# Decayed-attention stage of a fused attention and two-layer expert kernel: 64x64 array tiles for two products, a two-step state update, and two smaller moves

## The reference

```python
def _attn_ref(r, k, v, w, u) -> np.ndarray:
    B, H, S, D = r.shape                     # 4, 8, 768, 48
    state = np.zeros((B, H, D, D), dtype=np.float32)
    y = np.zeros_like(r)
    for t in range(S):
        kt, vt, rt = (k[:, :, t], v[:, :, t], r[:, :, t])
        cur = np.einsum('bhd,bhe->bhde', u[None] * kt, vt)
        y[:, :, t] = np.einsum('bhd,bhde->bhe', rt, state + cur)
        state = w[None, :, :, None] * state + np.einsum('bhd,bhe->bhde', kt, vt)
    return y.astype(np.float32)
...
    x = np.ascontiguousarray(attn_out.transpose(0, 2, 1, 3)).reshape(B * S, H * D)
    x = _moe_ref(x=x, **moe_kwargs)           # 8 experts, 384 of 3072 tokens each: relu(x @ w1[e]) @ w2[e]
    return _moe2_ref(x=x, **moe2_kwargs)      # relu(x @ w_in)**2 @ w_out, width 2048
```

## Time and profile before

| | us |
|---|---|
| median of 3 runs | 817.01 |
| lowest and highest of the runs | 812.26 and 819.65 |
| the profiled execution, as a run | 811.83 |
| its span in the profile | 810.1 |
| TensorE busy in the span | 775.9 (96%) |
| attention's units, TensorE: first `scores` to the last gate | 7.6 to 127.3 |

### The profile page before, as it was taken

One profiled execution on the slowest core, in us unless ns is written; L12 is line 12 of the kernel. 1 busy time (PEld: TensorE's weight loads), 2 busy tenths in 40 slices (PEclk: granted clock), 3 DMA queues, 4 the chain that ended last, 5 costly groups with the idle time before them and its releaser, 6 DMA issues.

```text
span 810.1 us, 19168 instructions
## 1 busy us (share of the span) xinstructions
PE 775.9 (96%) x6971; PEld 741.8 (92%) x6971; DVE 501.4 (62%) x1195; ACT 321.4 (40%) x718; POOL 293.5 (36%) x295
## 2 busy tenths in 40 slices
PE   7999995789999999999999999999999999999996
PEld 6999994589899999999999999999999999999995
DVE  7888886787846783678377837783777236721210
ACT  4555654223532353235323532353236324531332
POOL 8666640102631263126312631263126312621333
PEclk9999996699999999999999999999999999999999
DMA  8888744502300140013001300130013002300000
GB/s 215 240 257 242 230 141 177 167 18 77 110 1 30 48 137 0 29 54 131 0 29 57 128 0 29 57 127 0 29 59 125 0 30 79 108 1 30 0 1 30
DMA packets 22196, 65.27 MB, mean 81 GB/s; under 512 B 3664, under 2 KB 6736, under 8 KB 22160
## 3 DMA queue, kind: packets, MB, share of 16 engines
q1 hardware_dynamic: 19088, 55.34, 21.6%
q0 software_dynamic: 3072, 9.44, 3.3%
HBM read 55.33 MB, written 9.44 MB: 80 GB/s over the span
## 4 chain that ended last, share of the span: by engine, by line
PE 76%; DVE 12%; issue 5%; POOL 3%; ACT 2%; DMA 1%; POOLq 0%; DVEq 0%; SPq 0%; ACTq 0%
PE bank L1359 14%; PE bank L1363 14%; PE bank L1360 13%; PE bank L1417 7%; PE bank L1418 6%; PE bank L1419 6%; PE bank L1163 3%; PE bank L1201 3%; PE bank L1176 3%; DVE hot L860 2%; DVE hot L974 2%; PE bank L1230 1%; DVE sq L1073 1%; PE bank L1217 1%; POOL xg L473 1%
## 5 line engine op out<-in xcount | busy, mean ns | idle before, releaser
L500 POOL TENSOR_TENSOR h_lo<-sq,h_hi 128x384 fp32r<-128x384 f32 x128 | 155.4, 1217 | 375.7 <-DVE sq L1073 375.6
L1073 DVE SCALAR_TENSOR_TENSOR sq<-bank,relu 128x384 f32<-128x384 f32 x128 | 71.1, 555 | 150.4 <-ACT relu L624 148.4
L624 ACT ACTIVATE relu<-bank 128x384 f32<-128x384 f32 x128 | 62.9, 492 | 193.6 <-PE bank L1363 180.3
L1417 PE MATMUL bank<-m_hi,h_hi 128*128 128x384 f32 x384 | 132.2, 344 | 2.3 <-POOL h_lo L500 2.0
L1359 PE MATMUL bank<-x_hi,m_hi 128*128 128x384 f32 x384 | 129.6, 337 | 0.6
L1363 PE MATMUL bank<-x_hi,m_lo 128*128 128x384 f32 x384 | 130.0, 338 | 0.0
L1418 PE MATMUL bank<-m_lo,h_hi 128*128 128x384 f32 x384 | 129.6, 338 | 0.0
L1419 PE MATMUL bank<-m_hi,h_lo 128*128 128x384 f32 x384 | 129.2, 337 | 0.0
L1360 PE MATMUL bank<-x_lo,m_hi 128*128 128x384 f32 x384 | 128.8, 335 | 0.0
L618 ACT ACTIVATE h_hi<-bank 128x384 fp32r<-128x384 f32 x64 | 31.5, 492 | 175.4 <-PE bank L1363 175.4
L1065 DVE SCALAR_TENSOR_TENSOR h_lo<-bank,h_hi 128x384 fp32r<-128x384 f32 x64 | 35.5, 554 | 73.2 <-ACT h_hi L618 73.2
(11 more groups left out here) (191 smaller groups left out, 1446.5 us busy)
## 6 DMA issues: line engine op xcount, KB each, us to landing
w_raw<-we_in SPq DMA_DIRECT2D x48, 512.0 KB
nn<-nn_in SPq DMA_DIRECT2D x24, 384.0 KB, 3.9
tt<-tt_in SPq DMA_DIRECT2D x44, 192.0 KB, 4.3
m_raw<-m_in SPq DMA_DIRECT2D x12, 512.0 KB, 6.3
x_rows<-yrow SPq DMA_DIRECT2D x24, 192.0 KB, 2.4
tt<-tt_in SPq DMA_DIRECT2D x4, 256.0 KB, 5.7
xg<-x_rows,perm_next POOLq DMA_INDIRECT x24, 5.3
out<-xg,perm_now POOLq DMA_INDIRECT x24, 2.6
```

Source lines behind the costliest of these rows:

```text
L500: pool.tensor_tensor(h_lo[g % 3][:, :], sq[g % 2][:, :], h_hi[g % 3][:, :].bitcast(f32), ALU.subtract).then_inc(lo2_ready, 1)
L624: act.activation(relu[:, :], h_ps[g % 3][:, 0:CAP], ACT.Relu).then_inc(relu_ready, 1)
L1073: dve.scalar_tensor_tensor(out=sq[g % 2][:, :], in0=h_ps[g % 3][:, 0:CAP], scalar=0.0, in1=relu[:, :], op0=ALU.max, op1=ALU.mult).then_inc ...
L1417: pe.matmul(acc_ps[t][:, 0:DM], h_hi[r][:, s], m2_hi[:, c:c + DM], start=first, stop=False)
```

## The change

- `scores` and `inter` are cut by 64 also in the other direction: `scores` computes 64 columns of weights (64 of the 128 key steps) at a time into half of the partitions, and `inter` 64 of the 128 query steps. Each has 16 products where it had 8. `inter` streams 64 columns of the state where it streamed 128 (48 are used), and the padding of `state` shrinks with it. In front of both, TensorE raises a semaphore of its own (`pe_held`), so that the waits stand in its instruction stream ahead of the products and not in the first weight load.
- `state_sum` becomes one multiplication of the state by `w_chunk` into a new tile `faded`, which stands in front of the waits for `update_ready` and `inter_done`, and one addition of the PSUM result, which also waits for `faded_ready`.
- `in_high` rounds half a tile (512 columns) behind each of the last two units of a chunk; the semaphore counts two per tile, and the waits for it are doubled.
- GpSimd waits for `scaled` to reach 3 before it makes `rk` of unit 2, once.

```diff
-        state = [sb(f"state{b}", [HD, PAIRS * D + P - D], f32, att) for b in range(B)]
+        state = [sb(f"state{b}", [HD, PAIRS * D + HALF - D], f32, att) for b in range(B)]
+        faded = sb("faded", [HD, PAIRS * D], f32, att)
...
-                        sp.wait_ge(in_hi_ready, i + 1)
+                        sp.wait_ge(in_hi_ready, 2 * i + 2)
...
             def in_low(i, part):
-                pool.wait_ge(in_hi_ready, i + 1)
+                pool.wait_ge(in_hi_ready, 2 * i + 2)
...
+                    if is_first(i) and b == 0:
+
+                        pool.wait_ge(scaled, 3)
                     if not last or b < B - 2:
                         bonus(i + (b + 2) // B, (b + 2) % B)
...
-            def in_high(n):
+            def in_high(n, piece):
                 act.wait_ge(in_loaded, 16 * n + 16)
-                cols = bass.ds(n * WT, WT)
+                cols = bass.ds(n * WT + piece * (WT // 2), WT // 2)
...
-                    if not last and b == B - 1:
-                        in_high(i + 1)
+                    if not last and b >= B - 2:
+                        in_high(i + 1, b - B + 2)
...
             def state_sum(i, b):
                 n = 4 * i + b
+                dve.wait_ge(state_ready, n + B)
+                dve.tensor_tensor(faded[:, :].rearrange("p (q d) -> p q d", q=PAIRS),
+                                  state[b][:, 0:PAIRS * D].rearrange("p (q d) -> p q d", q=PAIRS),
+                                  w_chunk[:, :].unsqueeze(2).broadcast_to([HD, PAIRS, D]), ALU.mult).then_inc(faded_ready, 1)
                 dve.wait_ge(update_ready, n + 1)
                 dve.wait_ge(inter_done, n + 1)
-                for p in range(PAIRS):
-                    c = slice(p * D, (p + 1) * D)
-                    done = dve.scalar_tensor_tensor(out=state[b][:, c], in0=state[b][:, c], scalar=w_chunk[:, p:p + 1],
-                                                    in1=u_ps[0:HD, c], op0=ALU.mult, op1=ALU.add)
-                done.then_inc(state_ready, 1)
+                dve.wait_ge(faded_ready, n + 1)
+                dve.tensor_tensor(state[b][:, 0:PAIRS * D], faded[:, :], u_ps[0:HD, 0:PAIRS * D],
+                                  ALU.add).then_inc(state_ready, 1)
...
             def scores(i, b):
+                pe.sem_inc(pe_held, 1)
                 for p in range(PAIRS):
                     for a in range(2):
                         rows = slice(a * HALF, a * HALF + D)
-                        last = pe.matmul(sc_ps[a][:, p * P:(p + 1) * P], ks[rows, p, :], rs[j][rows, p, :], start=True, stop=True)
+                        for s in range(0, P, HALF):
+                            last = pe.matmul(sc_ps[a][s:s + HALF, p * P:(p + 1) * P], ks[rows, p, s:s + HALF], rs[j][rows, p, :],
+                                             start=True, stop=True)
...
             def inter(i, b):
+                pe.sem_inc(pe_held, 1)
                 for p in range(PAIRS):
                     for a in range(2):
                         rows = slice(a * HALF, a * HALF + D)
-                        last = pe.matmul(y_ps[j][:, a, p * P:(p + 1) * P], rs[j][rows, p, :], state[b][rows, p * D:p * D + P],
-                                         start=p == 0, stop=False)
+                        for t in range(0, P, HALF):
+                            last = pe.matmul(y_ps[j][t:t + HALF, a, p * P:p * P + HALF], rs[j][rows, p, t:t + HALF],
+                                             state[b][rows, p * D:p * D + HALF], start=p == 0, stop=False)
```

More of the change, by code:

```diff
@@ L244, in build @@
         rk_ready, own_made, ownv_ready = sem("rk_ready"), sem("own_made"), sem("ownv_ready")
-        kn_ready, state_ready = sem("kn_ready"), sem("state_ready")
+        kn_ready, state_ready, faded_ready = sem("kn_ready"), sem("state_ready"), sem("faded_ready")
         yT_sum, yT_ready, logit_sum, logit_ready = sem("yT_sum"), sem("yT_ready"), sem("logit_sum"), sem("logit_ready")
@@ L256, in build @@
         perm_kept = sem("perm_kept")
-        pool_held = sem("pool_held")
+        pool_held, pe_held = sem("pool_held"), sem("pe_held")
         gather_sent = sem("gather_sent")
@@ L577, in units @@
                         own_values(i + (b + 1) // B, (b + 1) % B)
-                    if not last and b == B - 1:
-                        in_high(i + 1)
+                    if not last and b >= B - 2:
+                        in_high(i + 1, b - B + 2)
             own_copy(0, 0)
             own_values(0, 0)
-            in_high(0)
+            in_high(0, 0)
+            in_high(0, 1)
             units(0, False)
```

## The result

| | before | after |
|---|---|---|
| median of 20 runs of each, us | 814.85 | 822.25 |
| lowest and highest, us | 811.34 and 822.68 | 816.22 and 835.06 |
| ratio after to before | | 1.0078 (95%: 1.0053 to 1.0102) |
| profiled execution, us, and its span | 811.8, 810.1 | 821.4, 819.6 |
| `scores` of unit 8 starts at, us | 47.39 | 58.29 |

The forecast was 810 in a range up to 820: wrong, and on the other side. The three stretches (+10.9, -3.7, +1.8 us) give 9.0 of the 9.5 us by which the spans differ. So the change won in the middle most of what was promised (0.29 us a unit for 0.36), and lost three times as much in the first eight units.

What follows compares the result with a forecast made beforehand. TensorE was taken as the bound, 4.745 us per unit going to 4.39. Start -1.0, 18 units -6.4, `pe_held` +0.5 and tail 0 gave -6.9 us: 817.0 - 7 = 810 us, range 801.5 to 820.

Steps and rivals of the forecast that it cites:

- the start: First units of the attention: `scores` of unit 3 starts earlier, -1.0 us in the sum, bounds -1.7 and 0.
- The tail: Last three units of the attention: TensorE alone would win 1.3 us, but VectorE enters late; taken as 0.
- Scores and inter in four tiles: TensorE's products: four tiles run at once, `inter` 0.45 us for 0.89, `scores` 1.06, saving 0.44 us per unit on `inter`.
- The slow rival: TensorE still runs only two tiles at a time: `scores` over 1.5 us, unit +0.9, total 834 us; chance 0.13.
- State sum: VectorE's `faded` stands behind GpSimd's `kn` in some units, making 4.39 us per unit; bounds 4.25 and 4.7.
- `pe_held`, "between 0 and 0.1 us per unit": Waits ahead of TensorE's products cost nothing when running ahead, a restart when `rs` is just in time; taken as 0.03.
- Weights in halves: ScalarE's halved weight copy no longer holds back `yT` in one unit of four: 0.05 us per unit, 0.9 us in all.
- rk of unit 2 later: GpSimd: `rs` of unit 2 takes 0.7 us instead of 2.44; after later meetings -1.0 us remains.
- DMA: Input transfers: same bytes in less time, share 0.90, inputs requested four units ahead; costed at nothing.
- The sum: Whole attention: start -1.0, 18 units -6.4, `pe_held` +0.5, last three units 0; together -6.9 us.
- The clock: Attention: a granted clock below full would show the forecast wrong; no sign of it seen, no chance given.

Runs made afterwards that it cites:

- e2: The changed kernel with the four old state operations in place of `faded` and the addition; 818.59 us, ratio 1.0033 to the kernel before.
- e13: e11 plus the change's two `pe_held` increments per unit on TensorE's queue, old tiles; 817.85 us, ratio 1.0001 to the kernel before.
- e8: The kernel before with only GpSimd's later `rk` of unit 2 added; 812.29 us, ratio 0.9966 to the kernel before.
- e12: The changed kernel without the later `rk` of unit 2; 822.18 us, ratio 1.0083 to the kernel before.
- e6: The changed kernel, but in the last chunk GpSimd waits for the unit's row sum before multiplying `rk`; 823.90 us, ratio 1.0066 to the kernel before.
- e1: The changed kernel with `scores` back to its old products, only `inter` in four tiles; 818.07 us, ratio 0.9991 to the kernel before.
- e17: The changed kernel without `pe_held`, each group's first product in old form, old state operations, old tiles in units 0 to 3; 827.04 us, ratio 1.0115.
- e14: e7 with the change's GpSimd order and `pe_held` only ahead of `inter`, from unit 4 on; 812.50 us, ratio 0.996 to the kernel before.
- e18: e14 with `scores` in four tiles too from unit 4 on, `pe_held` ahead of both; 814.14 us, ratio 0.9973 to the kernel before.
- e3: The changed kernel loading only a quarter of each input of units 4 to 23; 820.34 us, ratio 1.0034 to the kernel before.
- e11: e8 plus ScalarE's weight copies in two halves, all else old; 811.62 us, ratio 0.9942 to the kernel before.
- e4: The kernel before loading only a quarter of each input of units 4 to 23; 814.69 us, ratio 0.999 to the kernel before.
- e10: e8 plus the state sum as two operations (`faded`, addition), tiles unchanged; 815.37 us, ratio 0.999 to the kernel before.
- e7: The changed kernel with `scores` in halves, old tiles in units 0 to 3, old state operations, `rk` after the row sum in the last chunk; 815.76 us, ratio 0.9972.
- e9: e8 plus 64 bare semaphore increments per unit on TensorE's queue; 1108.86 us, ratio 1.3608 to the kernel before.
- e15: The changed kernel without `pe_held`, the first product of `scores` and of `inter` in old form; 832.22 us, ratio 1.0113 to the kernel before.

## Why the prediction was wrong, step by step

The step that failed is the start, -1.0 us in the sum: it measured +10.9. TensorE waited for its own program, which the prediction counted neither in bytes nor in time, and ran at half clock behind two of these waits. The tail, taken as 0, was +1.8.

- **Scores and inter in four tiles**: right in mechanism and size (0.46 and 1.03 to 1.10). The slow rival, two tiles at a time, did not come: `scores` never took over 1.2 us at full clock.
- **State sum**: right that `faded` meets `kn`, and 4.45 a unit for the forecast's 4.39. But e2 shows its price apart: 0.06 us, not the 0.14 that I had between 4.25 and 4.39. The rest of what stands above 4.22 is there without `faded`, because VectorE is late for `rs` then too. That the sum came out near is in part luck.
- **`pe_held`, "between 0 and 0.1 us per unit"**: right for a unit in steady state (0.04 in e13), wrong for the start, where it cost e13 7 us. I looked at whether the wait would be hidden, never at what an instruction of that kind costs the engine that issues it (0.14 us bare) or holds back behind it (the fetch of the next block).
- **Weights in halves**: 0.03 for 0.05 us a unit. Right.
- **rk of unit 2 later, "-1.0 us remains"**: right in size where it stood alone (e8: -1.28 at scores(3), -1.15 at scores(8)), worth nothing in the change (e12). The wait for `rs` until 18.83 us had covered the wait for the block of instruction 471, which with four tiles is reached at 14.5 and comes at 18.0. I named no work that hides behind a wait that I removed.
- **DMA, "I cost it at nothing"**: the inputs were indeed never late. But I counted only the bytes that the kernel moves, and the engines also move the program.
- **The sum**: it failed in its frame, "what the change can win is what these pieces lose, until another engine is late". The pieces say what the array does; 64 more instructions per unit come from outside. I had the count (16 products where there were 8) and the page's line on q8, and joined neither to a time. A block needed in 3.8 us against one in 5.4 before was to be had from rows of before; whether the supply would keep up was not, and that was the bound to give.
- **The clock, "for which there is no sign"**: it was named as what would make the forecast wrong, with no chance of its own. Half of the loss at the start, and about half of that at the end, is half clock behind a standstill.
- **The tail, "I take 0"**: +1.8, `rs` behind `rk` at the loop's end, where GpSimd has no `kn` to keep it back. e6 gave 2.9 us back.

Shown: the stops lie at borders of 256 instructions, only where the program is new, and each ends 1.2 to 1.6 us behind a packet of q8 (all traces); fewer instructions shorten or remove them (e1, e17, e14 against e18, where the tiles change with the count); a lighter load on the DMA engines brings the blocks of the first pass sooner (e3); `pe_held` alone makes one (e13 against e11), by a packet that starts 1.6 us later; data waits without such a stop can halve the clock too (e4). Open: why the packet starts later with `pe_held`, as only its time is known, and what decides whether a stop costs the clock. Behind stops of 2.34 (before), 1.99 (e6, at 56.28 us), 1.92 (e10) and 1.62 us (e12, at 47.16 us) it stayed full; it fell during or within 2.4 us behind stops of 0.70 (e17), 0.91 (e1, at 47.02 us), 1.27 (e7), 1.54 (e13) and 1.60 (e18), so length alone does not tell.

## What to carry to other kernels

Count instructions as well as microseconds: where an engine's program is new and the DMA engines are busy, compare the time in which it would use 256 of them with the spacing of the packets on the instruction queue, and put denser forms only into code that repeats. When a change takes a wait away, ask what else was waiting under it, and look at all waits of a microsecond and more at TensorE twice, since the clock may charge for them again. Try the small parts alone: here two lines and the halves made 0.6% faster (e11), while the large part, which did in the array what it should, made the whole 0.8% slower.

## What the runs showed of the hardware

- TensorE's program came in packets of 16 KB, one per 4.1 to 5.9 us beside a DMA share of 0.5 to 0.75, one per 4.1 to 4.7 us at about 0.35 (e3); needed sooner, TensorE stood for 0.4 to 3.3 us per packet, and went on 1.2 to 1.6 us behind its end.
- A packet started 1.6 us later where `pe_held` stood in front of `scores` in the old tiling (17.15 us in e13, 15.58 in e11).
- A bare semaphore increment on TensorE's queue took 0.14 us (64 in 8.85, e9).
- Four 64x64 tiles ran at once in float32, as far as the times tell: `inter`, 32 records of 64 columns, in 0.46 us. Changing between 128-wide and 64-wide tiles cost about 0.2 us, an estimate from e15 (0.41 us for one wide product among small ones); `inter` behind 128-wide `scores` took 0.62 us for 0.46 (e7).
- A VectorE operation with two SBUF inputs stood for as long as GpSimd worked on end: 4.60 us for 0.68 (e4), 2.81 for 0.34 (e10).
